# Attention: grams and scores of groups 2 to 5 from one product, buffers and loads dealt anew

## The reference

```python
k_n = k / (norm(k) + 1e-6);  state = 0
for t in range(768):
    y[t] = q[t] @ state
    v_old = state^T k_n[t]
    state = state + beta[t] * outer(k_n[t], v[t] - v_old)
```

## Time and profile before

| | us |
|---|---|
| median of 3 runs | 887.62 (880.94 to 888.03) |
| the profiled execution | 886.0 |
| its span, first to last instruction | 884.2 |
| TensorE busy in the span | 826.7 (93%) |
| VectorE / ScalarE / GpSimd busy | 473.2 / 294.2 / 198.3 |
| mean granted clock of TensorE | 0.946 |

### The profile page before, as it was taken

One profiled execution on the slowest core, in us unless ns is written; L12 is line 12 of the kernel. 1 busy time (PEld: TensorE's weight loads), 2 busy tenths in 40 slices (PEclk: granted clock), 3 DMA queues, 4 the chain that ended last, 5 costly groups with the idle time before them and its releaser, 6 DMA issues.

```text
span 884.2 us, 24719 instructions
## 1 busy us (share of the span) xinstructions
PE 826.7 (93%) x10634; PEld 801.1 (91%) x10634; DVE 473.2 (54%) x1076; ACT 294.2 (33%) x658; POOL 198.3 (22%) x173
## 2 busy tenths in 40 slices
PE   7588899899887999999999999999899999999998
PEld 7478889898876999999999999999799899899898
DVE  5999999999467834434434442333741431431421
ACT  5245665666342121112211221122531421421412
POOL 2123123043006506200710000000222222222221
PEclk9658987899796999999999999999999999999999
DMA  6724544423481210210002003003311010000001
GB/s 205 204 71 123 146 137 141 119 84 85 145 271 62 75 52 19 67 53 24 18 18 71 0 18 119 19 19 116 141 54 36 18 53 36 18 0 36 19 1 54
DMA packets 38171, 65.15 MB, mean 74 GB/s; under 512 B 4345, under 2 KB 26178, under 8 KB 38082
## 3 DMA queue, kind: packets, MB, share of 16 engines
q1 hardware_dynamic: 38082, 63.85, 23.3%
HBM read 46.66 MB, written 14.16 MB: 69 GB/s over the span
## 4 chain that ended last, share of the span: by engine, by line
PE 61%; issue 21%; DVE 12%; POOL 2%; ACT 2%; DMA 1%; SPq 0%; POOLq 0%; DVEq 0%; ACTq 0%
PE m_ps_h L1189 12%; PE g_ps_v L1690 11%; PE m_ps_d L1174 11%; PE ps_ga L450 3%; PE g_ps_y L1690 3%; PE ps_y L536 3%; DVE prod L618 3%; PE ps_r L501 3%; PE ps_y L541 3%; DVE t_lane L622 2%; PE ps_u L519 2%; POOL g_vn_lo L1587 2%; PE ps_s L554 2%; PE g_ps_u L1690 2%; PE ps_ga L475 2%
## 5 line engine op out<-in xcount | busy, mean ns | idle before, releaser
L1374 DVE SCALAR_TENSOR_TENSOR m_h_lo<-m_ps_h,m_h_hi 128x512 fp32r<-128x512 f32 x72 | 49.6, 690 | 101.8 <-ACT m_h_hi L1051 101.8
L1174 PE MATMUL m_ps_d<-m_w_hi,m_h_hi 128*128 128x384 f32 x288 | 97.6, 339 | 0.0
L1174 PE MATMUL m_ps_d<-m_w_hi,m_h_lo 128*128 128x384 f32 x288 | 96.4, 335 | 0.0
L1174 PE MATMUL m_ps_d<-m_w_lo,m_h_hi 128*128 128x384 f32 x288 | 96.3, 334 | 0.0
L1051 ACT ACTIVATE m_h_hi<-m_ps_h 128x512 fp32r<-128x512 f32 x72 | 43.0, 597 | 151.6 <-PE m_ps_h L1189 151.6
L450 PE MATMUL ps_ga<-kq 64*64 64x64 f32 x1536 | 60.2, 236 | 18.9 <-DVE t_lane L622 10.7
L1189 PE MATMUL m_ps_h<-m_unt_hi,m_w_hi 128*128 128x256 f32 x432 | 75.7, 285 | 2.2 <-DVE m_h_lo L1374 1.3
L450 PEld LDWEIGHTS ps_ga<-kq 64*64 64x64 f32 x1536 | 56.7, 151 | 19.9 <-DVE t_lane L622 10.8
L1189 PE MATMUL m_ps_h<-m_unt_hi,m_w_lo 128*128 128x256 f32 x432 | 74.7, 282 | 0.0
L1189 PE MATMUL m_ps_h<-m_unt_lo,m_w_hi 128*128 128x256 f32 x432 | 74.7, 282 | 0.0
L618 DVE TENSOR_TENSOR prod<-g_lane,t_lane 128x31 f32<-128x31 f32 (+15 forms) x186 | 69.6, 374 | 6.2
(11 more groups left out here) (223 smaller groups left out, 1928.0 us busy)
## 6 DMA issues: line engine op xcount, KB each, us to landing
kq<-kq_g SPq DMA_DIRECT2D x48, 256.0 KB, 3.5
v_in<-v_g SPq DMA_DIRECT2D x12, 384.0 KB, 3.3
k_in<-k_g SPq DMA_DIRECT2D x12, 384.0 KB, 3.2
x_scr<-y_sb SPq DMA_DIRECT2D x24, 192.0 KB, 3.6
stage<-w_ch SPq DMA_DIRECT2D x6, 768.0 KB, 6.2
x_scr<-m_x_sb SPq DMA_DIRECT2D x24, 192.0 KB, 1.9
g_x<-x_scr SPq DMA_DIRECT2D x24, 192.0 KB, 4.5
out<-g_y SPq DMA_DIRECT2D x24, 192.0 KB, 1.9
```

The source lines that it names most:

```text
L1174: last = pe.matmul(out, first[x], second[y], start=(k == 0 and m == 0), stop=(k == n - 1 and m == 2))
L1374: dve.scalar_tensor_tensor(h_lo[:, 2 * g:2 * g + 2].rearrange("p f t -> p (f t)"), ps_h[g % 2][:, :], 0.0, h_hi[:, 2 * g:2 * g + 2].rearra ...
```

## The change

- A product `both(g, p)` of keys with keys and queries together, 4 units in 8 matmuls of 64 x 128 columns, takes the place of a gram piece and a score piece for groups 2 to 5. ScalarE takes its bank with two copies of 256 columns. Eight of them make a group.
- In the scan, group 3's are made in steps 4 to 7 of group 0, two a step; group 4's in steps 6, 7 of group 1 and 0, 1 of group 2; group 5's in steps 6, 7 of group 2 and 0, 1 of group 3. So groups 0 to 4 have 8, 4, 8, 4 and 0 of them, where they had 4, 6, 7, 4 and 3 pieces (two pieces are the columns of two `both`).
- `gram_sb` has three buffers for four, `score` four for three.
- Loads of `kq`: group 3's all in steps 0 to 3, the others' keys and queries by turns. `diagonal` stands in steps 1, 0, 2, 2 of groups 0 to 3 for 0, 1, 1, 1; `roots` in step 6 of each for 6, 5, 4, 4.
- ScalarE copies y before the state in each step.

```diff
--- before.py
+++ after.py
@@ -42,24 +42,28 @@
     TINY = 2.0 ** -100
     LINKS = 2 * (H - 1) + 2
     AHEAD = 24
-    ROOT_STEP = (6, 5, 4, 4)
+    ROOT_STEP = (6, 6, 6, 6)
+    DIAG_STEP = (1, 0, 2, 2)
     WARM = 42
     PARTS = ((1, 0, 16), (2, 16, 24), (3, 24, 32))
     assert U == 32 and PR == 4 and x_scr.shape[0] == NB
 
-    FIRST = (("g", 0), ("a", 0), ("g", 1), ("a", 1), ("g", 2), ("a", 2))
-    PIECES = {(0, 5): "g30", (0, 6): "g31", (0, 7): "g32 g33",
-              (1, 2): "a30", (1, 3): "a31", (1, 4): "a32", (1, 5): "g40", (1, 6): "g41", (1, 7): "g42",
-              (2, 0): "g43", (2, 1): "a33", (2, 3): "a40", (2, 4): "a41", (2, 5): "g50", (2, 6): "g51", (2, 7): "g52",
-              (3, 0): "g53", (3, 1): "a42", (3, 3): "a43", (3, 5): "a50",
-              (4, 0): "a51", (4, 1): "a52", (4, 2): "a53"}
-    assert G == 6
+    FIRST = (("g", 0), ("a", 0), ("g", 1), ("a", 1))
+    assert G >= 3
     uses = [(what, g, p) for what, g in FIRST for p in range(4)]
+    uses += [("b", 2, p) for p in range(N)]
     uses += [("w", 0, 0), ("x", 0, 0)]
 
+    def both_at(i, n):
+
+        if i == 0:
+            return [(3, n - 4)] if n >= 4 and G > 3 else []
+        if n >= N - 2:
+            return [(i + 3, n - N + 2)] if i + 3 < G else []
+        return [(i + 2, n + 2)] if n < 2 and i >= 2 and i + 2 < G else []
+
     def pieces_at(i, n):
-
-        return [(x[0], int(x[1]), int(x[2])) for x in PIECES.get((i, n), "").split()]
+        return [("b", g, 2 * q + h) for g, q in both_at(i, n) for h in range(2)]
 
     for k in range(STEPS):
         i, n = k // N, k % N
@@ -82,17 +86,18 @@
             return sems.enter_context(nc.semaphore(name))
 
         kq = [None] * 4
-        gram_sb, score, k_in, v_in, tt = [None] * 4, [None] * 3, [None] * 2, [None] * 2, [None] * 2
+        gram_sb, score, k_in, v_in, tt = [None] * 3, [None] * 4, [None] * 2, [None] * 2, [None] * 2
 
         def group_buffers(p):
-            score[p + 1] = sb(f"score{p + 1}", [P, U, C])
+            score[p] = sb(f"score{p}", [P, U, C])
             k_in[p], v_in[p] = sb(f"k_in{p}", [P, U, D]), sb(f"v_in{p}", [P, U, D])
             tt[p] = sb(f"tt{p}", [P, U, C])
 
         for p in (2, 3):
             kq[p] = sb(f"kq{p}", [P, 2, U, C])
-        for p in range(4):
+        for p in range(3):
             gram_sb[p] = sb(f"gram_sb{p}", [P, 2, U, H])
+        score[3] = sb("score3", [P, U, C])
         g_diag = sb("g_diag", [P, U, H])
         g_lane = [sb(f"g_lane{p}", [P, H, H]) for p in range(2)]
         t_lane = sb("t_lane", [P, H, H])
@@ -115,7 +120,7 @@
         u_sb = sb("u_sb", [P, 2, PR, D])
         s_sb = sb("s_sb", [P, NB, PR, D])
         y_sb = sb("y_sb", [P, NB, PR, 2, D])
-        score[0] = sb("score0", [P, U, C])
+        score[2] = sb("score2", [P, U, C])
         kq[0] = sb("kq0", [P, 2, U, C])
         group_buffers(0)
 
@@ -195,10 +200,10 @@
                              y_sb[:, b].rearrange("p r h e -> p (r h e)")).then_inc(y_out[b], 16)
 
             def diagonal(g):
-                sp.wait_ge(ga_out, turn["g", g, 3] + 1)
+                sp.wait_ge(ga_out, turn["b", g, N - 1] + 1 if g >= 2 else turn["g", g, 3] + 1)
                 sp.wait_ge(glane_ok, g)
                 for a in range(4):
-                    sp.dma_start(g_diag[quarter(a)], gram_sb[g % 4][quarter(a), a % 2]).then_inc(diag_in, 16)
+                    sp.dma_start(g_diag[quarter(a)], gram_sb[g % 3][quarter(a), a % 2]).then_inc(diag_in, 16)
 
             for p in range(4):
                 load_kq(0, 0, p)
@@ -228,18 +233,21 @@
                     sp.wait_ge(u_ok, k)
                 if g and n < NB - 1:
                     results(g - 1, n + 1)
-                if n == (1 if g else 0) and two:
+                if two and n == DIAG_STEP[g]:
                     diagonal(g + 2)
-                if n == 3 and three:
-                    if g:
-                        sp.wait_ge(y_done, N * g)
+                if g == 0 and n < 4 and three:
+                    load_kq(3, 0, n)
+                    load_kq(3, 1, n)
+                if g and n == 3 and three:
+                    sp.wait_ge(y_done, N * g)
                     load_kq(g + 3, 0, 0)
-                if n == 4 and three:
-                    load_kq(g + 3, 0, 1)
-                if n == 5 and three:
+                if g and n in (4, 5) and three:
+                    load_kq(g + 3, 1, n - 4)
+                if g and n == 6 and three:
+                    load_kq(g + 3, 0, 2)
+                if g and n == 7 and three:
                     load_kq(g + 3, 0, 3)
-                if n in (6, 7) and three:
-                    load_kq(g + 3, 1, 2 * n - 12)
+                    load_kq(g + 3, 1, 3)
                 if 2 <= k <= STEPS - NB:
                     sp.wait_ge(y_ok, k - 1)
                 if n in (0, 2) and g + 1 < G:
@@ -250,10 +258,10 @@
                     if g and n == 3:
                         sp.wait_ge(s_done, N * g)
                     load_k(g + 1, n // 4)
-                if n == 4 and three:
-                    load_kq(g + 3, 0, 2)
-                if n in (6, 7) and three:
-                    load_kq(g + 3, 1, 2 * n - 11)
+                if g and n == 4 and three:
+                    load_kq(g + 3, 0, 1)
+                if g and n == 6 and three:
+                    load_kq(g + 3, 1, 2)
                 if n == N - 1 and g + 1 < G:
                     results(g, 0)
                 for load in ahead.get(k - N * (G - 1), ()):
@@ -265,8 +273,8 @@
 
         def gpsimd(pool, tokens_clear):
             def causal(g, p):
-                pool.wait_ge(ga_out, turn["a", g, p] + 1)
-                a = score[g % 3][:, QU * p:QU * p + QU]
+                pool.wait_ge(ga_out, turn["a", g, p] + 1 if g < 2 else turn["b", g, 2 * p + 1] + 1)
+                a = score[g % 4][:, QU * p:QU * p + QU]
                 later = mask[:, ::-1] if g >= G // 2 else mask[:]
                 pool.tensor_tensor(a, a, later.unsqueeze(1).broadcast_to([P, QU, C]), ALU.mult).then_inc(masked, 1)
 
@@ -341,12 +349,21 @@
                 act.wait_ge(ga_done, m + 1)
                 us = slice(QU * p, QU * p + QU)
                 if what == "g":
-                    act.activation(gram_sb[g % 4][:, :, us].rearrange("p b u s -> p u b s"),
+                    act.activation(gram_sb[g % 3][:, :, us].rearrange("p b u s -> p u b s"),
                                    ps_ga[m % 2][:, :].rearrange("p (u b s) -> p u b s", b=2, s=H),
                                    ACT.Copy).then_inc(ga_out, 1)
                 else:
-                    act.activation(score[g % 3][:, us].rearrange("p u t -> p (u t)"), ps_ga[m % 2][:, :],
+                    act.activation(score[g % 4][:, us].rearrange("p u t -> p (u t)"), ps_ga[m % 2][:, :],
                                    ACT.Copy).then_inc(ga_out, 1)
+
+            def both(g, p):
+                m = turn["b", g, p]
+                act.wait_ge(ga_done, m + 1)
+                us = units(p)
+                act.activation(gram_sb[g % 3][:, :, us].rearrange("p b u s -> p u b s"),
+                               ps_ga[m % 2][:, :].rearrange("p (u k b s) -> p u k b s", k=2, b=2, s=H)[:, :, 0], ACT.Copy)
+                act.activation(score[g % 4][:, us], ps_ga[m % 2][:, :].rearrange("p (u k t) -> p u k t", k=2, t=C)[:, :, 1],
+                               ACT.Copy).then_inc(ga_out, 1)
 
             def solved_w(g, c):
                 m = turn["w", g, c]
@@ -386,8 +403,10 @@
                     piece(what, g, p)
                     if (what, g, p) == ("a", 0, 1):
                         roots(0)
-                    if (what, g, p) == ("a", 2, 1):
-                        roots(1)
+            for p in range(N):
+                both(2, p)
+                if p == 5:
+                    roots(1)
             solved_w(0, 0)
             corners(0, 0)
             solved_x(0, 0)
@@ -408,9 +427,6 @@
                 if k >= 2:
                     j = k - 2
                     b, c = j % NB, (j // NB) % 2
-                    if j < STEPS - NB:
-                        act.wait_ge(s_done, j + 1)
-                        act.activation(s_sb[:, b], state(b, slice(0, P)), ACT.Copy).then_inc(s_ok, 1)
                     act.wait_ge(y_done, j + 1)
                     if j >= N:
                         act.wait_ge(y_out[b], 16 * (j // N))
@@ -418,10 +434,14 @@
                     act.activation(y_sb[rows, b].rearrange("p r h e -> p h r e"),
                                    ps_y[rows].rearrange("p (h x) -> p h x", h=2)[:, :, 0:PR * D].rearrange(
                                        "p h (r e) -> p h r e", e=D), ACT.Copy, scale=-1.0).then_inc(y_ok, 1)
+                    if j < STEPS - NB:
+                        act.wait_ge(s_done, j + 1)
+                        act.activation(s_sb[:, b], state(b, slice(0, P)), ACT.Copy).then_inc(s_ok, 1)
                 if k >= STEPS:
                     continue
```

(27 more changed lines are left out.)

## The result

| | before | after |
|---|---|---|
| median of 20 runs, us | 886.48 (880.94 to 891.92) | 882.13 (878.44 to 886.42) |
| ratio of the runs, 95% interval | | 0.9947 (0.9927 to 0.9966) |
| span of the profiled execution, us | 884.2 | 881.4 |

The changed kernel is faster by 0.5%, 4.4 us. I had forecast 1.1 us more than before. The time lies in the range, near rival A's 883.1, and "within 1%" was right; but the direction was wrong.

A forecast was written before the change was run, and what follows sets the result against it. VectorE's inverses, about 34 us each, were the floor; TensorE lost mostly clock. Late inverses +1.1, y order -1.0 and last group's clock +1.0 gave +1.1 on 886.0, 887.1; the median lies 1.6 above: 888.7 us, range 880.5 to 895.5.

The forecast's parts named there:

- rival A: Whole kernel: group 3 starts by 152.5, nothing is late and VectorE's floor is met; 883.1 us, chance 0.27.
- Last group's clock: Group 5: TensorE waits about 6 us at its start, slow time becomes 15.4 for 13.4; +1.0 us (-1.6 to +3.6).
- y order: Scan steps: copying y before the state gives back 0 to 0.2 us a step, about 1.0 us in group 5.
- VectorE is a floor, and what is saved becomes idle time: Attention: inverses of about 34 us each set a line that no TensorE saving lowers; TensorE waits instead.
- The new piece, 0.90 us: TensorE's products: 8 matmuls of 128 columns take 0.90 us against 0.94 for the old piece, 1.3 us saved over 32.
- Rival C: Wide products are dear: 1.09 us a piece makes group 2 1.5 us longer; 890.2 us, chance 0.10.
- Group 0 loses its slow stretch, group 1 ends at 109.5 and waits 4.5: TensorE's 3.05 us idle after group 0 goes, likely with the slow stretch (5.2 us); group 1 then waits for the inverse at 114.0.
- Group 3 starts at 154.0: Start of group 3's coupling: between 152.5 and 155.9, taken as 154.0 against 156.5 before.
- roots(4) late by 1.4: Group 2: roots moved to step 6 end at 151.1, so VectorE waits 1.4 us (0 to 3.3).
- diagonal(5): Group 3: diagonal issued at 170.0 lands at 174.8 against 173.56 needed; bounds none to 5.5 us late.
- v(4): Group 3: its late load let GpSimd's scaling hold a VectorE link for 2.73 us; forecast to stay.
- B: Rival: u of step 2 in group 3 ready after 168.8, each us then costs VectorE one; 894.7 us, chance 0.18.

The follow-up runs named there:

- the steps back: Changed kernel with roots of group 4 back in step 4 and diagonal of group 5 back in step 1: 879.96 us, ratio 0.9894; again 880.63, 0.9927.
- two products: Changed kernel with each product of 128 columns made as two of 64: 885.87 us, ratio 1.0016 to the kernel before.
- filler: Changed kernel with the steps back, unused products filling TensorE's last-group waits ahead of w and x: 880.7 us, 0.9924; ahead of w alone: 885.09, 0.9985.
- the copy order alone: Kernel before with one edit, ScalarE copying y before the state in every step: 882.99 us against 885.37, ratio 0.9966.

## Why the prediction was wrong

**The step that failed is the last term, "Last group's clock": +1.0 us.** It was of the wrong sign. It took two lengths of slow stretch from elsewhere, 15.4 in the mean, and set them against 13.4; the stretch at the head of group 5 came out at 13.7, so the length was near. What I left out is where it lies, and the idle time. TensorE's wait starts the stretch, at 218.0, 5.8 us before x, and so a good part of it slows nothing. Behind x that is 2.1 us gained, and 2.6 us more came from idle time in the instruction stream, which stood in no term. That 4.7 us against a term of 1.0 loss and 1.0 gain (the y order) is nearly the whole error of this pair, -4.7 where I had 0; x itself came 0.8 us later by the change, where I had 1.1. The split of one pair is partly chance: the mean over the profiles above gives half of 6.5 us for the clock and 1.6 for the gaps. And 1.1 us of the distance between 888.7 and 882.13 is the start of the sum: the kernel before has a median of 886.48 over 20 runs, not 887.62.

Step by step:

- *VectorE is a floor, and what is saved becomes idle time:* right. TensorE waited 4.5 us for it at group 5 and 0.5 ahead of x, near the 6 I had; at group 4 it waited 2.1, which I had not.
- *The new piece, 0.90 us:* two took 1.90 and 1.77 us, 0.95 and 0.88. Rival C is not borne out. The rule of "TensorE: Matmul & The Clock Gate", section "Back-to-back issue gap", in the Trainium skill, by which I had estimated 1.05 us, is not borne out by the trace either: 128 columns cost here about twice what 64 cost, not 2.2 times. Its worth was mis-sized, though: undoing it in the changed kernel costs 0.7%, 6 us (2.8 at the near ends of the intervals), where I had 1.3. With the steps back it is 2 to 5 us, and the intervals overlap. What carries it is only read from traces: the diagonal over its edge, and gaps from 50 to 262 us of 13.5 and 16.6 us with two products, against 9.2 to 14.7 with one (without filler).
- *Group 0 loses its slow stretch, group 1 ends at 109.5 and waits 4.5:* wrong. With the wait gone no stretch began at 80, but one came at 91.7, behind a gap of 0.84 us, for 10.2 us, and group 1 ended at 115.0, with the inverse; TensorE waited 0.14 us. The removed wait put the stretch off and did not end it: the other profiles in which TensorE waited less than 0.7 us there have one of 3.4 to 10.2 us that starts between 90 and 96.
- *Group 3 starts at 154.0:* 153.8 here, but 148.9 to 154.9 over the profiles of kernels with wide products. The agreement is partly chance: group 2 began 1.1 us later than I had and took 1.3 less.
- *roots(4) late by 1.4:* not seen. ScalarE made it at 150.19, and VectorE took it at 151.30; no wait. *diagonal(5):* 1.7 us in one profile, none in the other. At the last group +0.8 us, forecast +1.1; the number held, partly by luck, since half of the lateness of the inverses came from v of group 3 and the wait for the diagonal was in part made up by a shorter link beside v(4), which I had said would stay. Its upper bound, 5.5, was passed only by the kernel with two products (6.0).
- *y order, 1.0 us in group 5:* alone it is worth 3.0 us (0.9 to 5.1), so 1.0 is just inside. The mechanism was right, 0.2 us a step; the size is too small by the middle value, and the other groups may gain too: in one profile group 3 starts 3.2 us earlier with it.
- *The rivals:* A (883.1) is nearest to the median and had 0.27; one profile has its mechanism up to group 5, the other the forecast's late diagonal with a gain all the same. B's condition, u of step 2 after 168.8, was just met (SP went on at 169.92), its price was not.

Open: whether the late diagonal costs the median anything. Unpaired the steps back look like 0.5% (0.9894 against 0.9947), paired 0.1%, and both intervals overlap. Open too is which instruction packet brings a gap and which does not (last section).

## What to carry to other kernels

Before pricing a slow stretch, ask what TensorE does during it: one that passes while the engine waits for another anyway is nearly free, and here a wait at the head of a stage that TensorE bounds brought it forward. Count instructions beside columns: half the matmuls of twice the width saved 0.1 us a pair of pieces, yet undoing them cost the changed kernel 6 us. When steps race against an inverse with slack of 1 to 2 us, a single profile decides nothing; the same program was late in one and on time in another.

## What the hardware showed that I had not expected

TensorE's "issue" waits from 50 to 262 us add up to 14.4 us before, 10.5 after and 9.2 to 19.1 over the other kernels. They go with the instruction packets of 16 KB. Each of the 18 gaps before and of the 17 after ends 2.2 to 3.1 us after such a packet starts, while packets come some 4 us apart; in the trace of before, for instance, packets start at 158.37, 198.11 and 222.17, and gaps end at 160.53, 200.75 and 224.51. Fewer instructions mean fewer packets (69 before, 65 after). The five profiles with narrow products have 13.5 to 19.1 us of gaps, the eight with wide ones and no filler 9.2 to 14.7. That fewer packets lower the idle time fits this, but the ranges overlap, and the kernels differ in more. "Runtime: NRT & Kernel Launch" in the Trainium skill, section "Instruction fetch mechanics", has instructions fetched in blocks of 16 KiB, 256 each; the traces agree (994 instructions fewer, 4 packets fewer). It also has the fetch hidden behind the issue of instructions; there the traces differ, if these gaps are the fetch.

The clock fell to 1.2 GHz during or behind idle times of very different length: for 10.2 us behind 0.84 us of it, 13.7 us about a wait of 4.5 us, 10.2 us in the trace with two products behind a gap of 1.50 us, and 20.5 us in the kernel with the copy order alone behind one of 1.43 us. In the last two TensorE was busy for all of the stretch. So the length of the idle time just before says little about how long the slow time lasts.
